# Reordering the work behind the last expert of a two-layer mixture of experts, and converting weights in the middle of a step

## The chip, the cores and the metric

The kernel runs on one core of a Trainium2 chip. The metric is the device time of one execution in microseconds (us). Matrix products run on TensorE (PE), copies out of PSUM and conversions on ScalarE (ACT) and VectorE (DVE), gathers and scatters are issued by GpSimd (POOL), and plain DMAs by SyncE (SP). Each engine works through its own instructions in order, and waits for others on semaphores.

## The reference

Three stages follow each other: attention with 4 sink keys and a window of 128, a first mixture of experts in which each of 1536 tokens goes to 2 of 8 experts, and a second one in which each token goes to one expert. Only the end of the first and the second are touched here:

```python
e_idx = np.argmax(logits, axis=1)          # logits = x @ w_gate + modality_bias[modality_id]
gate_w = probs[np.arange(N), e_idx]
for e in range(E):                         # E = 8 experts, N = 1536, D = 512, F = 1024
    mask = e_idx == e
    h = np.maximum(x[mask] @ w1[e], 0.0)
    out[mask] = gate_w[mask, None] * (h @ w2[e])
```

Everything is float32.

## The kernel before

**Precision.** Each float32 operand of the large products is split into a high part (written as fp32r) and a low part (the rest). ACT writes the high part by a copy, DVE the low part by a subtraction, and PE adds three products: high x high, high x low, low x high. The weights of an expert are 4 chunks of 128 x 2048 (1 MB each): chunks 0 and 1 are w1, 2 and 3 are w2. `split` has two slots for the two parts of an expert's weights.

**First layer, its end.** Expert 7 is the last of the first layer. Behind its products PE computes the scores of the second router for the tokens that expert 7 touches (`last_logits`, which needs yT of all four `y1_copy` of ACT), turns the output back to rows (`back`, 4 subtiles k = 0 to 3) and adds the scores to the tokens (`last_to_tokens`, which needs `last_share` of DVE). ACT scales the rows (`last_scale`), POOL scatters them (`scatter1`).

**Second router.** DVE picks each token's expert (`pick`), PE counts (`ranks(1)`), DVE places the tokens (`second_places`, `second_hots`), PE turns the places into lists of tokens (`codes2`), DVE reads them out (`second_sources`). `chosen_gate` on DVE, `coded_tiles(1)` and `coded_gates` on POOL, `slot_gates` on PE and again on DVE yield the gate of each row. `expert_order` writes the order in which experts are loaded, `tile_owners` and `fresh_tiles` which expert each tile has, and in which step new weights are to be converted (`todo`).

**Second layer.** Tokens are taken in tiles of 128. The most popular expert is known early, from 8 of the 12 blocks of 128 tokens: its weights come into `stage` (`popular_high`, `popular_low`, chunk by chunk), and tiles 0 and 1 are filled with its tokens, before the rest of the router is done. For tile t PE does `tx(t)` (turn x), `first(t, half)` twice (x @ w1), `th(t, half)` twice (turn h), and `second(t)` in two halves (h @ w2). ACT does `x_high`, `relu`, `h_high`; DVE `x_low`, `h_low`, and `y_copy` (times gate); POOL `gather` and `scatter`. A half of `first` or `second` is 8 matmuls of 512 columns with the high part of x or h, and 4 with the low part, which wait for `x_low` or `h_low` alone. `second_weights` converts the second expert; it comes through `raw`, loaded by SP when `order_ready` is 3.

**The loop.** From tile 3 on all engines go through `step(t)`: PE does first(t) with th(t-1) between, tx(t+1), second(t-1). `next_weights(t)` converts chunks 0 and 1 of the next expert in the first tile's step of an expert, and chunks 2 and 3 one step later. With these inputs the second layer has 14 tiles and 3 experts in use: tiles 0 to 6, tile 7, and tiles 8 to 13. Only steps 7 and 8 convert.

All order is written out by hand: the calls stand in each engine's program in the order in which it executes them.

## Time and profile before

| | us |
|---|---|
| median of 3 runs | 677.1 (675.16 to 678.22) |
| profiled execution | 675.41 |
| its span | 673.6 |
| PE busy in the span | 638.2 |
| PE busy from 463.7 us to the end of the span | 183.7 |
| PE's granted clock, mean over the span | 0.985 |

The span runs from the first to the last recorded instruction. A row of a timeline gives the start, the busy time, the engine, the line of the program, the operation, what it writes and reads, and in brackets how long the engine stood idle just before and what released it. "issue" means that the profile shows nothing that it waited for. A granted clock of 1.00 is 2.4 GHz, and 0.50 is 1.2 GHz. Busy matmuls overlap, so that the start of the next one, not the end of the last, tells the pace.

### The profile page before, as it was taken

The numbers are of one execution on the slowest core, as the hardware profiler recorded it, in microseconds if no ns is written. First come the engines' busy times: TensorE is split into PE (matmuls) and PEld (weight loads), VectorE is DVE, ScalarE is ACT, GpSimd is POOL, SyncE is SP. The second block draws the span as 40 slices with busy tenths as digits, with TensorE's granted clock in tenths as the row PEclk, the third lists the DMA queues.
The fourth block names the chain that finished last, engine by engine and source line by source line (L and its number), as shares of the span: only waits on it lengthen the run. The fifth ranks groups of instructions, "written<-read, shape, count | busy, mean of one in ns | idle before, by whom it ended". The sixth has DMA issues, their size and how long they took to land.

```text
span 673.6 us, 11243 instructions
## 1 busy us (share of the span) xinstructions
PE 638.2 (95%) x3866; PEld 580.5 (86%) x3867; DVE 328.5 (49%) x681; ACT 276.0 (41%) x529; POOL 185.1 (27%) x199
## 2 busy tenths in 40 slices
PE   7989999899999999999999999997989999999981
PEld 6989999898999999999999999986767888788861
DVE  4466645587465527263462624467767222542220
ACT  5668866442444234243433523234526123522110
POOL 2500100117361533516153241102542121121010
PEclk8999999999999999999999999999899999999996
DMA  7877822263684645646364510615549211011000
GB/s 209 280 245 245 284 71 73 70 245 79 231 231 132 139 128 157 190 145 165 108 127 161 156 20 12 162 63 172 157 165 369 92 48 47 20 33 47 16 32 11
DMA packets 51089, 89.84 MB, mean 133 GB/s; under 512 B 7919, under 2 KB 14063, under 8 KB 51040
## 3 DMA queue, kind: packets, MB, share of 16 engines
q1 hardware_dynamic: 41872, 69.21, 30.7%
q0 software_dynamic: 9168, 19.97, 13.4%
q8 instruction: 31, 0.51, 0.3%
q14 instruction: 18, 0.15, 0.1%
HBM read 73.13 MB, written 17.02 MB: 134 GB/s over the span
## 4 chain that ended last, share of the span: by engine, by line
PE 83%; DVE 6%; DMA 3%; issue 2%; ACT 2%; SPq 1%; POOL 0%; ACTq 0%; DVEq 0%; POOLq 0%
PE banks L1061 6%; PE banks L1060 6%; PE banks L1000 6%; PE banks L1079 6%; PE banks L1002 6%; PE banks L999 6%; PE banks L804 5%; PE banks L832 4%; PE banks L1343 4%; PE banks L1344 4%; PE banks L1348 4%; PE banks L1371 3%; PE banks L1372 3%; PE banks L1375 3%; PE banks L816 2%
## 5 line engine op out<-in xcount | busy, mean ns | idle before, releaser
L1825 DVE TENSOR_TENSOR split<-stage,split 128x2048 fp32r<-128x2048 f32 x32 | 73.3, 2290 | 41.6 <-ACT split L1455 41.4
L999 PE MATMUL banks<-xTs,split 128*128 128x416 f32 (+1 forms) x256 | 88.6, 350 | 0.0
L1000 PE MATMUL banks<-xTs,split 128*128 128x416 f32 (+1 forms) x256 | 86.4, 342 | 0.0
L651 POOL DMA_INDIRECT x_moe<-rows,dst_idx x25 | 49.3, 1971 | 113.2 <-DVE rows L2277 112.2
L1060 PE MATMUL banks<-hTs,split 128*128 128x416 f32 x224 | 79.9, 357 | 0.0
L1061 PE MATMUL banks<-hTs,split 128*128 128x416 f32 x224 | 78.6, 351 | 0.0
L1590 ACT ACTIVATE hTs<-banks 128x416 fp32r<-128x416 f32 x56 | 29.0, 518 | 81.5 <-PE banks L1002 81.5
L1455 ACT ACTIVATE split<-stage 128x2048 fp32r<-128x2048 f32 x32 | 61.0, 1908 | 0.7 <-DMA stage<-w1a 0.7
L1713 ACT ACTIVATE hTs<-banks 128x512 fp32r<-128x512 f32 x28 | 16.5, 597 | 105.3 <-PE banks L1358 105.3
L1002 PE MATMUL banks<-xTs,split 128*128 128x416 f32 (+1 forms) x256 | 56.2, 340 | 0.0
L1835 DVE CUSTOM_DVE_ANT_0 negs<-banks,masks 128x260 f32<-128x260 f32 (+2 forms) x96 | 34.9, 402 | 36.3 <-PE banks L804 35.1
L804 PE MATMUL banks<-k_sb,q_sb 128*128 128x260 f32 (+2 forms) x192 | 49.1, 380 | 3.6 <-DMA k_sb<-k_w 1.8
L1988 DVE SCALAR_TENSOR_TENSOR hTs<-banks,hTs 128x416 fp32r<-128x416 f32 x56 | 32.8, 587 | 38.7 <-ACT hTs L1590 38.7
L749 POOL DMA_INDIRECT out<-rows,dst x14 | 14.2, 1012 | 128.6 <-DVE rows L2430 111.5
L1343 PE MATMUL banks<-split,xTs 128*128 (+1 forms) x112 | 45.9, 410 | 3.6 <-issue 2.0
L1468 ACT ACTIVATE probs<-negs,negmax 128x260 f32<-128x260 f32 (+2 forms) x96 | 46.1, 484 | 7.2 <-DVE negmax L1835 7.2
L999 PEld LDWEIGHTS banks<-xTs,split 128*128 128x128 f32 x256 | 48.2, 188 | 0.7 <-issue 0.3
L1371 PE MATMUL banks<-split,hTs 128*128 (+1 forms) x112 | 45.3, 404 | 3.5 <-DVE rows L2430 1.8
L1000 PEld LDWEIGHTS banks<-xTs,split 128*128 128x128 f32 x256 | 48.2, 188 | 0.3
L1079 PE MATMUL banks<-hTs,split 128*128 128x416 f32 x224 | 48.0, 356 | 0.0
L2249 DVE TENSOR_TENSOR xTs<-banks,xTs 128x512 fp32r<-128x512 f32 (+1 forms) x28 | 16.4, 590 | 64.2 <-ACT xTs L1559 64.2
L1002 PEld LDWEIGHTS banks<-xTs,split 128*128 128x128 f32 x256 | 46.3, 188 | 0.3
(371 smaller groups left out, 1308.8 us busy)
## 6 DMA issues: line engine op xcount, KB each, us to landing
stage<-w1a SPq DMA_DIRECT2D x16, 1024.0 KB, 5.8
stage<-w2a SPq DMA_DIRECT2D x16, 1024.0 KB, 5.5
k_sb<-k_w SPq DMA_DIRECT2D x12, 520.0 KB, 4.8
raw<-w1b SPq DMA_DIRECT2D x4, 1024.0 KB, 6.4
raw<-w2b SPq DMA_DIRECT2D x4, 1024.0 KB, 9.5
q_sb<-q_t SPq DMA_DIRECT2D x24, 128.0 KB, 3.4
x_attention<-rows SPq DMA_DIRECT2D x12, 256.0 KB, 6.3
split<-x_moe SPq DMA_DIRECT2D x12, 256.0 KB, 3.7
```

The costliest lines, as they stand in the source:

```text
L651: pool.indirect_dma_start(out=x_dram[1], out_offset=rows_at(dst_idx[0], early_dst, e, k), in_=y_lines(e, k), in_offset=None, compute_op=AL ...
L804: mm = pe.matmul(S[:, j % 2, h, 0:n], q_sb[:, b, pair, h, :], k_sb[:, b, pair, 0:n], start=True, stop=True)
L999: pe.matmul(psum, piece(slot, 0, o + c * FH), xTs[:, 0, c, 0:cols], start=(c == 0), stop=False)
L1000: pe.matmul(psum, piece(slot, 1, o + c * FH), xTs[:, 0, c, 0:cols], start=False, stop=False)
L1002: mm = pe.matmul(psum, piece(slot, 0, o + c * FH), xTs[:, 1, c, 0:cols], start=False, stop=(c == DC - 1))
L1060: pe.matmul(psum, piece(e % 2, 0, o), hTs[:, 0, c, 0:cols], start=(c == 0), stop=False)
L1061: pe.matmul(psum, piece(e % 2, 1, o), hTs[:, 0, c, 0:cols], start=False, stop=False)
L1079: mm = pe.matmul(psum, piece(e % 2, 0, DC * F + c * D + d * P), hTs[:, 1, c, 0:cols], start=False, stop=(c == FC - 1))
L1343: pe.matmul(psH[:, half, :], xTs2[:, 0, c, :], weights(slot, 0, o), start=(c == 0), stop=False)
L1371: pe.matmul(psY, hTs2[:, 0, c, :], weights(slot, 0, o), start=(c == 0), stop=False)
L1455: act.activation(split_chunk(e % 2, 0, c), staged_chunk(e % 2, c), ACT.Copy).then_inc(high_done[c], 1)
L1825: dve.tensor_tensor(split_chunk(e % 2, 1, c), staged_chunk(e % 2, c), split_chunk(e % 2, 0, c).bitcast(F32), ALU.subtract).then_inc(low_do ...
```

## The change

One wait of SP goes, `codes2` moves into second(0), and the calls behind expert 7 stand in another order on PE, ACT and DVE. In the loop `next_weights(t)` stands between the two halves instead of at the end. No computation is added or left out.

```diff
@@ SP, load of the second expert
             sp.wait_ge(last_added, 1)
-            sp.wait_ge(gathered[0], 32)
             for c in range(CHUNKS):
@@ PE, second(t, e, slot)
-                        if isinstance(t, int) and t == 1 and half == 1:
-                            tx(2, 0, 2)
+                        if isinstance(t, int) and half == 1:
+                            if t == 0:
+                                codes2()
+                            elif t == 1:
+                                tx(2, 0, 2)
@@ PE, second_layer
                 tx(0, 0, 1)
                 back(last, 2, banks[:, 3, :])
+                first(0, 0, 0, 1)
                 back(last, 3, banks[:, 4, :])
-                first(0, 0, 0, 1)
-                ranks(1)
-                pe.wait_ge(scaled1, nth_sub(E, 0))
+                pe.wait_ge(scaled1, nth_sub(last, 0) + 1)
                 first(0, 1, 0, 1)
                 tx(1, 1, 1)
+                ranks(1)
                 first(1, 0, 0, 1)
+                pe.wait_ge(scaled1, nth_sub(E, 0))
                 th(0, 0)
                 first(1, 1, 0, 1)
-                codes2()
                 th(0, 1)
                 second(0, 0, 1)
                 slot_gates()
@@
-                e, slot = expert(2)
-                first(2, 0, e, slot)
-                first(2, 1, e, slot)
+                e2, slot2 = expert(2)
+                first(2, 0, e2, slot2)
+                first(2, 1, e2, slot2)
                 tx(3, 1, 2)
-                step(3, 1, 3)
+                th(2, 0)
+                e3, slot3 = expert(3)
+                first(3, 0, e3, slot3)
+                first(3, 1, e3, slot3)
+                th(2, 1)
+                tx(4, 0, 3)
+                second(2, e2, slot2)
@@ ACT, end of the first layer
                 turned_copy(2)
-                popular_high(0)
                 y1_copy(last, 3)
@@ ACT, step
                     h_high(t - 1, 0)
                     relu(t, 0)
+                    next_weights(t)
                     h_high(t - 1, 1)
                     relu(t, 1)
@@
-                    next_weights(t)
@@ DVE, step
                     h_low(t - 1, 0)
+                    next_weights(t)
                     h_low(t - 1, 1)
@@
-                    next_weights(t)
                     y_copy(t - 1, 1 - b, went)
@@ DVE, expert_phase
-                popular_low(0)
                 popular_first()
                 last_share()
-                popular_low(1)
+                popular_low(0)
                 late_scores()
                 all_scores()
+                x_low(0)
+                popular_low(1)
                 pick(noisy, 0, chosen[:], done_key)
...
-                x_low(0)
+                chosen_gate()
+                popular_low(2)
+                x_low(1)
                 second_places()
-                x_low(1)
-                chosen_gate()
                 second_hots()
-                popular_low(2)
-                second_sources()
                 h_low(0, 0)
                 popular_low(3)
+                second_sources()
                 h_low(0, 1)
+                slot_gates()
+                y_copy(0, 0, 0)
                 expert_order()
+                h_low(1, 0)
+                h_low(1, 1)
                 tile_owners()
                 fresh_tiles()
-                slot_gates()
-                y_copy(0, 0, 0)
-                h_low(1, 0)
-                h_low(1, 1)
                 x_low(2)
+                y_copy(1, 1, 0)
                 second_weights((0, 1))
-                y_copy(1, 1, 0)
                 x_low(3)
```

The start of ACT's part is shown by its instructions. On ACT, from the end of expert 7 on, before (`split<-stage1` is popular_high, `yT<-banks` y1_copy(last,3), `raw<-banks,sub_gate` last_scale, `xTs2<-banks` x_high, `rows<-banks` relu, `rc<-rb` the Exp):

```order
L1693 ACTIVATE split<-stage1 128x2048
L1596 ACTIVATE yT<-banks 128x416
L1693 ACTIVATE split<-stage1 128x2048
L1628 ACTIVATE raw<-banks,sub_gate 128x512 x2
L1702 ACTIVATE xTs2<-banks 128x512
L1628 ACTIVATE raw<-banks,sub_gate 128x512 x2
L1693 ACTIVATE split<-stage1 128x2048
L1708 ACTIVATE rows<-banks 128x512
L1693 ACTIVATE split<-stage1 128x2048
L1708 ACTIVATE rows<-banks 128x512
L1770 ACTIVATE rc<-rb 128x96
L1702 ACTIVATE xTs2<-banks 128x512
```

The same place of ACT now:

```order
L1604 ACTIVATE yT<-banks 128x416
L1700 ACTIVATE split<-stage1 128x2048 x2
L1636 ACTIVATE raw<-banks,sub_gate 128x512 x2
L1709 ACTIVATE xTs2<-banks 128x512
L1636 ACTIVATE raw<-banks,sub_gate 128x512
L1715 ACTIVATE rows<-banks 128x512
L1636 ACTIVATE raw<-banks,sub_gate 128x512
L1700 ACTIVATE split<-stage1 128x2048
L1776 ACTIVATE rc<-rb 128x96
L1715 ACTIVATE rows<-banks 128x512
L1709 ACTIVATE xTs2<-banks 128x512
L1700 ACTIVATE split<-stage1 128x2048
```

The copy of yT has moved ahead of the first popular_high, and x_high(1) ahead of the last one; between relu(0,0) and relu(0,1) stand now popular_high(2) and the Exp.

On DVE, around the gates of the rows, before (`used`, `tile_expert` end tile_owners, `last_used` to `todo` are fresh_tiles, the next three rows slot_gates, `rows<-banks,slot_gate` y_copy(0), `hTs` h_low(1,0) and (1,1)):

```order
L2118 TENSOR_SCALAR used<-noise_sb 128x1
L2119 CAST tile_expert<-owner_f 128x21
L2134 TENSOR_SCALAR last_used<-noise_sb 128x1
L2135 MEMSET shared 128x2
L2136 TENSOR_TENSOR shared<-owner_f 128x19
L2137 SCALAR_TENSOR_TENSOR shared<-owner_f,last_used,shared 128x19
L2139 SCALAR_TENSOR_TENSOR todo<-shared 128x20
L2202 COPY shared<-banks 128x63
L2204 TENSOR_TENSOR shared<-shared 128x21
L2205 TENSOR_TENSOR slot_gate<-shared 128x21
L2430 TENSOR_SCALAR rows<-banks,slot_gate 128x512
L2422 TENSOR_TENSOR hTs<-banks,hTs 128x512 x2
```

The same place of DVE now (`noise_sb<-pair_up_to` to `order` are expert_order):

```order
L2210 COPY shared<-banks 128x63
L2212 TENSOR_TENSOR shared<-shared 128x21
L2213 TENSOR_TENSOR slot_gate<-shared 128x21
L2438 TENSOR_SCALAR rows<-banks,slot_gate 128x512
L2110 TENSOR_REDUCE noise_sb<-pair_up_to 128x2
L2111 CAST used<-noise_sb 128x1
L2113 TENSOR_TENSOR noise_sb<-pair,iota_row 128x8
L2114 SCALAR_TENSOR_TENSOR pair_sq<-iota_row,pair_up_to 128x64
L2115 TENSOR_TENSOR pair_sq<-pair_sq,noise_sb 128x64
L2116 TENSOR_REDUCE order_f<-pair_sq 128x8
L2117 CAST order<-order_f 128x7
L2430 TENSOR_TENSOR hTs<-banks,hTs 128x512 x2
```

y_copy(0) now comes ahead of the order table, and the table ahead of h_low(1,0) and (1,1); the owners of the tiles come behind these.

## Rows read from the trace of the kernel before

**Rows 1.** The page: busy time of the engines in the whole span.
```profile
PE 638.2 (95%) x3866; PEld 580.5 (86%) x3867; DVE 328.5 (49%) x681; ACT 276.0 (41%) x529; POOL 185.1 (27%) x199
```

**Rows 2.** Timeline of PE to 483 us: start, busy, instruction, [idle before <-releaser].
```profile
466.26 1.06 PE L1139 MATMUL banks<-wg,yT 128*128 128x8 f32 x8 [1.62 <-ACT yT L1596]
...
470.44 1.44 PE L1149 MATMUL banks<-chosen,last_hot 128*128 128x24 bf16 x48 [1.75 <-DVEq L2344]
...
474.17 0.78 PE L1343 MATMUL banks<-split,xTs 128*128 128x512 f32 x1
...
482.85 0.47 PE L1343 MATMUL banks<-split,xTs 128*128 128x512 f32 x1 [0.96 <-issue]
```

**Rows 3.** Timeline of PE from 493 us to the step of tile 3.
```profile
493.99 0.50 PE L1371 MATMUL banks<-split,hTs 128*128 128x512 f32 x1 [1.00 <-DVE split L2408]
...
500.12 0.50 PE L1371 MATMUL banks<-split,hTs 128*128 128x512 f32 x1 [1.78 <-DVE rows L2430]
...
506.18 0.39 PE L1343 MATMUL banks<-split,xTs 128*128 x1
...
508.90 0.39 PE L1343 MATMUL banks<-split,xTs 128*128 x1
...
513.30 0.50 PE L1343 MATMUL banks<-split,xTs 128*128 x1 [1.08 <-issue]
```

**Rows 4.** Timeline of PE, steps of tiles 7 and 8.
```profile
572.20 0.39 PE L1371 MATMUL banks<-split,hTs 128*128 x1
...
576.66 0.49 PE L1343 MATMUL banks<-split,xTs 128*128 x1 [1.57 <-DVE split L1821]
```

**Rows 5.** Stretches: start:end, length, busy us (x instructions) per engine, clock, DMA share, GB/s.
```profile
470.00:475.50 5.50, 5.06 (x63) 4.90 (x64) 4.95 (x13) 2.22 (x4) 4.18 (x3) 0.50 0.88 299
```

**Rows 6.** Timeline of ACT behind expert 7.
```profile
463.89 1.91 ACT L1693 ACTIVATE split<-stage 128x2048 fp32r<-128x2048 f32 x1 [1.22 <-DMA stage<-w1b]
...
466.58 1.91 ACT L1693 ACTIVATE split<-stage 128x2048 fp32r<-128x2048 f32 x1 [0.38 <-DMA stage<-w1b]
468.40 1.25 ACT L1628 ACTIVATE raw<-banks,sub_gate 128x512 f32<-128x512 f32 x2
```

**Rows 7.** Timeline of SP: two loads of weights.
```profile
468.87 0.93 SPq L362 DMA_DIRECT2D stage<-w2b  x2
497.48 0.94 SPq L362 DMA_DIRECT2D raw<-w1b  x2
```

**Rows 8.** The tile stage, 455 to 500 us.
```profile
DMA to landing us min/median/max: 5.1/5.6/10.2
```

**Rows 9.** Timeline of DVE: the second router and y_copy(0).
```profile
478.30 0.26 DVE L2078 TENSOR_TENSOR counts<-banks,step 128x96 f32<-128x96 f32 x1 [1.59 <-PE banks L959]
...
481.28 0.42 DVE L2093 TENSOR_TENSOR xT<-tile_i,iota_row 128x252 f32<-128x252 int32 x1
...
484.26 1.77 DVE L2097 TENSOR_TENSOR row_hot<-row_i,iota_row 128x1536 bf16<-128x1536 int32 x1 [0.15 <-DVE gate L2241]
...
495.92 0.17 DVE L2109 CAST order<-order_f 128x7 int32<-128x7 f32 x1
...
499.31 0.75 DVE L2430 TENSOR_SCALAR rows<-banks,slot_gate 128x512 f32<-128x512 f32 x1
```

**Rows 10.** Timeline of ACT: chunk 1 of the second expert.
```profile
506.73 1.92 ACT L1450 ACTIVATE split<-raw 128x2048 fp32r<-128x2048 f32 x1 [0.71 <-DMA raw<-w1b]
```

**Rows 11.** Timeline of POOL.
```profile
484.50 1.60 POOL L716 TENSOR_TENSOR gate_rest<-gate,gate_parts 128x12 f32<-128x12 f32 x1
...
490.80 1.04 POOL L733 DMA_INDIRECT rows<-x_moe,src_idx  x1 [0.15 <-issue]
```

**Rows 12.** Timeline of ACT, the step of tile 7.
```profile
566.48 0.59 ACT L1708 ACTIVATE rows<-banks 128x512 f32<-128x512 f32 x1
...
571.54 3.72 ACT L1450 ACTIVATE split<-raw 128x2048 f32 x2 [0.77 <-issue]
```

**Rows 13.** Timeline of DVE, the step of tile 7.
```profile
573.84 4.49 DVE L1821 TENSOR_TENSOR split<-raw,split 128x2048 f32 x2 [2.35 <-ACT split L1450]
```

More of the change, by code:

```diff
@@ L1757, in second_weights @@
                         high_part(1, c)
+                popular_high(0)
                 popular_high(1)
@@ L1763, in expert_phase @@
                 last_scale(2)
+                relu(0, 0)
                 last_scale(3)
                 popular_high(2)
-                relu(0, 0)
-                popular_high(3)
-                relu(0, 1)
                 act.wait_ge(act_route, 6)
                 act.activation(rc[:], rb[:], ACT.Exp).then_inc(act_route, 1)
+                relu(0, 1)
                 x_high(1)
-                parted_tiles()
+                popular_high(3)
                 relu(1, 0)
                 h_high(0, 0)
+                parted_tiles()
                 relu(1, 1)
```

## The prediction, made before the result was known

> **What bounds the kernel now.** I read the page first, then PE's timeline behind 463.7 us, then the queues that its gaps point to. PE is busy 638.2 us of a span of 673.6 [rows 1], so time can only come from its gaps and from stretches at the lower clock. All edits act behind 463.7 us. There PE stands still 1.62 us for a copy of yT, 1.75 us for last_share, 0.96 us before first(1,0) [rows 2], 1.00 us for the low part of chunk 3, 1.78 us for y_copy(0), 1.08 us before first(3,0) [rows 3] and 1.57 us in the loop, before first(8,0) [rows 4]. From 470 to 475.5 us PE has a granted clock of 0.50 [rows 5], the 1.2 GHz level; it fell behind the first gaps.
>
> A half product (12 matmuls of 512 columns) takes 508.90 - 506.18 = 2.72 us at full clock [rows 3]: 1.8 for the first eight, 0.9 for the last four. Four transposes take some 0.35 us by PE's own order.
>
> **Up to first(0,0).** y1_copy(last,3) now goes ahead of popular_high(0), which held it from 463.89 for 1.91 us [rows 6]: the 1.62 us go. DVE does popular_first while PE is still busy and last_share ahead of popular_low(0), so the 1.75 us go as well. But PE doesn't keep that. ACT's second popular_high waits for its DMA until 466.58 in any order; 1.9 us for it and 1.25 for two last_scale end at 469.65 [rows 6], x_high(0) at 470.2, and first(0,0) starts at 470.3 instead of 474.17 [rows 2]: 3.9 us earlier, with a new wait of about 1.6 us in front.
>
> **Up to second(0).** If the clock stays at full, first(0,0), back(3), first(0,1), tx(1) and ranks end at 470.3 + 2.8 + 0.4 + 2.8 + 0.35 + 0.7 = 477.4. ACT has put popular_high(2), the Exp and relu(0,1) ahead of x_high(1). Chunk 2 is issued at 468.87 [rows 7] and lands after 5.6 us [rows 8], at 474.5; 1.9 + 0.2 + 0.5 + 0.6 later, at 477.7, first(1,0) starts instead of 482.85 [rows 2], 5.1 us earlier. Its last four matmuls wait for x_low(1), which stands on DVE behind chosen_gate (0.75) and popular_low(2) (2.2) from 476.6: 480.3, a new wait of 0.7. So th(0,0) comes at 481.2 and second(0) at 484.8, 4.8 us earlier. Its second half needs popular_low(3). On DVE 3.4 us of second_places (478.30 to 481.28 + 0.42), 1.8 of second_hots [rows 9], h_low(0,0) and the 2.2 of popular_low(3) follow on 480.2: 488.3, and the half starts there instead of 493.99 [rows 3], 5.6 us earlier. codes2 in the middle of second(0) costs nothing of its own, since it fills that wait. Chunk 3 lands 10.2 us after 469.4 [rows 7, 8], at 479.6, and is converted before relu(1,0) needs ACT at 481.8; up to 482 it is free.
>
> **Up to first(2,0).** slot_gates is reached at 491.4. y_copy(0) no longer stands behind expert_order, tile_owners and fresh_tiles: 0.65 us for the gates and 0.75 for the copy [rows 9] release second(1) at 493.5 instead of 500.12 [rows 3], 6.6 us earlier. h_low(1,0) stands behind expert_order and costs 0.4 of that. first(2,0) starts at 500.1 instead of 506.18: 6.1 us earlier.
>
> **The new wait.** This lead is not kept. The order table that releases the second expert's load is written at 495.92 + 0.17 = 496.1 before [rows 9], and at 493.4 + 1.7 = 495.1 now, one microsecond earlier. SP issued 1.4 us behind it, at 497.48 [rows 7], and ACT had chunk 1 at 506.73, 9.25 us after that [rows 10]. The removed wait on gathered[0] is worth nothing before, as that gather was issued at 490.80 [rows 11]; I take it at nothing (0 to 0.7 us, what it would have cost behind a table at 495.1). Now the issue is at 496.5, chunk 1 lands at 505.8, its conversion ends at 507.7, and behind it in ACT's queue stand relu(2,0), relu(2,1) and x_high(3). PE, which has th(2,0) behind tx(3), gets there at 505.9 and waits 2.4 us. first(3,0) starts at 509.5 instead of 513.30 [rows 3]. With th(2,0) already done, step 3 is 0.35 us shorter, of which I count 0.2: **-4.0 us** at first(4,0).
>
> **The loop.** Only tiles 7 and 8 convert in the loop. In step 7 ACT ends relu(7,0) at 567.1 and now converts there: 0.77 + 3.72 us [rows 12], to 571.6, h_high(6,1) to 572.1, just in time for the half at 572.20 [rows 4]. DVE's two low parts (4.49 us, [rows 13]) end at 574.3 and h_low(6,1) at 575.0, where PE's last four matmuls wanted it at 572.20 + 1.8 = 574.0: a wait of 0.95. It replaces the 1.57 (with its 0.2 of queue time, 0.75 gained). Step 8 has the same geometry and had no wait: 0.95 lost. Sum **+0.2 us**. Bounds: 0.75 + 0 if DVE gets in between, -0.8 us; twice the whole 4.49 without the 1.57, +7.4 us, if nothing covered a low part. I take +0.2, worked from the rows of this very step.
>
> **Sum.** -4.0 + 0.2 = -3.8 us on a profiled execution of 675.4 us (span 673.6): 671.6. That execution is 1.7 us under the median of 677.1 us, so the median comes to **673.3 us**.
>
> **A rule against it.** POOL's small subtractions took 1.60 us from 484.50 [rows 11], to 486.10, while DVE's row_hot ran from 484.26 to 486.03 [rows 9]. The change puts row_hot right behind the one-hots that POOL waits for, and popular_low(3) over its subtractions. By the rows I shift the end of coded_gates from 490.7 to 491.2, in time for slot_gates. The Trainium skill, SBUF — State Buffer, section "SBUF: two separate sides", says that a DVE operation with two SBUF inputs and a GpSimd operation that reads SBUF hold the shared ports in turn, each for its whole length. The trace agrees for the pair above, where the POOL operation ends 0.07 us behind the DVE one. With 0.1 to 0.5 us lost the rule leaves the sum as it is; where every POOL step meets a long DVE operation it gives the second rival below.
>
> **Rivals.**
> 1. The clock still falls (16%). For it: it fell once behind gaps of 1.62 and 1.75 us, and a gap of 1.6 stays. Against: the gaps of 1.00 and 1.78 us around 495 [rows 3] left it at full. If it is halved for 6.5 us behind 470, as before, the products end 3 us later, the order table with them: gain 0.8, 676.3 us.
> 2. POOL is held (12%). A third and fourth operation behind DVE, 2 us more, delays slot_gates and with it y_copy(0) and the order table by 1.4: 674.7 us.
> 3. The mid-step conversion costs nothing, or the load comes sooner (15%): first(8,0) 0.75 earlier and no loss in step 8, a gain of 4.8 to 5.5: 672.0 us.
> 4. Slower (9%): the second expert's chunk 1 is late. ACT's queue has the relu of tile 2 behind it, and PE now has th(2,0) directly behind tx(3), so each us of delay is one of the kernel's. It decides from a landing at 505.8 + 3.8 = 509.6 us on; 4 us beyond that, with the load sharing the engines with gathers and scatters that now come earlier, is 681 us. Against: the load before had the DMA engines just as full, and took 9.25 us.
>
> **Numbers.** The forecast has 48%, its own range is 672 to 675. A measurement of this kernel can tell about 0.5%, 3.4 us, so the line to faster is 673.7 us, 0.4 above the forecast. Of the forecast's 48, 30 lie beyond it and 18 within; the third rival adds 15 to faster, the first and second 28 to the same; the fourth 9 to slower. Faster 0.45, same 0.46, slower 0.09. The range for 8 in 10 reaches from the third rival to the first, with a us of the runs' own spread below: 670.8 to 677.0 us.
>
> **What would show it.** Right: no gap at last_logits(3); a wait of 1.6 us before first(0,0) near 470.3; clock at full through 470 to 476; first(2,0) near 500; a wait of over 2 us of th(2,0) for ACT behind chunk 1; first(3,0) near 509.5; in steps 7 and 8 waits of 0.95 us in front of the last four matmuls of second. Wrong: a clock of 0.50 behind 470, first(1,0) later than 479 (then chunk 2 was late), slot_gates waiting for POOL, or no wait at th(2,0), which would make it a gain of 6.

## The result, and the profile after

The changed kernel takes 679.43 us (median of 20 runs, 675.97 to 683.59), the kernel before 676.81 us on the same chip (20 runs). The ratio is 1.0039, 95% interval 1.0024 to 1.0055: slower by 0.4%, 2.6 us. I had forecast 673.3 us, a gain. The profiled execution took 679.85 us.

The page's busy time of PE, to set beside [rows 1]: the span is 677.9 us now instead of 673.6, and PE is busy 2.5 us more for the same products.

```profile
PE 640.7 (95%) x3866; PEld 579.3 (85%) x3867; DVE 329.9 (49%) x681; ACT 275.6 (41%) x529; POOL 185.1 (27%) x199
```

**Ahead of the loop.** PE's timeline after, to set beside [rows 2, 3]:

```profile
467.84 1.35 PE L1148 MATMUL banks<-chosen,last_hot 128*128 128x24 bf16 x48 [0.18 <-DVEq L2352]
...
471.08 0.47 PE L1342 MATMUL banks<-split,xTs 128*128 128x512 f32 x1 [0.97 <-ACT xTs L1709]
...
509.54 0.66 PE L1357 MATMUL banks<-ident,rows 128*128 128x128 f32 x4 [1.13 <-ACT rows L1715]
510.85 0.49 PE L1342 MATMUL banks<-split,xTs 128*128 x1 [0.66 <-ACT xTs L1709]
```

The 1.62 us for yT are gone and the 1.75 us before L1148 are 0.18. The new waits stand where they were forecast, but shorter: 0.97 us before first(0,0) instead of 1.6, 1.13 us before th(2,0) instead of 2.4. The executions differ before the change begins (by 0.76 us here), so I count from one mark in each: the start of the eight small products `banks<-early_moving,row_hot_popular`, at 461.88 us before and 462.64 after. From there first(4,0) starts after 63.87 us before and 60.13 after: **3.74 us gained**, where 4.0 were forecast.

**In the loop.** From first(4,0) to the end of the span it is 147.85 us before and 155.13 after: **7.28 us lost**, where 0.2 were forecast. All of it lies in the steps of tiles 7, 8 and 9, which last 14.03 + 12.42 + 12.40 = 38.85 us before and 15.57 + 16.63 + 14.11 = 46.31 after. PE's gaps there, after; before, the 1.57 us of [rows 4] was the only one over 0.25 us:

```profile
569.70 0.49 PE L1373 MATMUL banks<-split,hTs 128*128 x1 [0.32 <-ACT hTs L1720]
...
572.70 1.19 PE L1377 MATMUL banks<-split,hTs 128*128 x4 [0.92 <-DVE hTs L2430]
575.22 0.79 PE L1342 MATMUL banks<-split,xTs 128*128 x1 [1.33 <-issue]
...
586.77 0.49 PE L1373 MATMUL banks<-split,hTs 128*128 x1 [0.21 <-ACT hTs L1720]
...
589.83 1.19 PE L1377 MATMUL banks<-split,hTs 128*128 x4 [0.97 <-DVE hTs L2430]
591.85 0.67 PE L1342 MATMUL banks<-split,xTs 128*128 x1 [0.84 <-issue]
```

The two waits for DVE (L1377, the last four products of a second layer) are the 0.95 us that I forecast for each step, to within 0.03. What I did not forecast stands behind each: 1.33 and 0.84 us at the start of the next step that end in "issue", and in the column PEclk of the stretches (columns as in [rows 5]) the clock at its lower level:

```profile
574.00:576.00 2.00, 0.78 (x2) 0.69 (x3) 0.75 (x1) 0.00 (x0) 0.09 (x1) 0.73 0.00 0
576.00:578.00 2.00, 2.00 (x7) 1.52 (x6) 0.00 (x0) 0.00 (x0) 1.20 (x3) 0.50 0.11 38
578.00:580.00 2.00, 2.00 (x12) 1.63 (x11) 0.00 (x0) 0.00 (x0) 1.12 (x2) 0.91 0.19 47
...
593.00:595.00 2.00, 2.00 (x6) 1.54 (x6) 0.00 (x0) 0.00 (x0) 1.21 (x3) 0.50 0.03 3
```

The timelines of ACT and of DVE in step 7, to set beside [rows 12, 13]:

```profile
565.26 3.72 ACT L1458 ACTIVATE split<-raw 128x2048 f32 x2 [1.16 <-issue]
```

```profile
567.54 4.49 DVE L1829 TENSOR_TENSOR split<-raw,split 128x2048 f32 x2 [3.21 <-ACT split L1458]
571.96 0.68 DVE L2430 TENSOR_TENSOR hTs<-banks,hTs 128x512 fp32r<-128x512 f32 x1
```

The conversion ends on DVE at 572.0, and h_low(6,1) is queued behind it.

**POOL.** The two small casts of coded_gates, and what DVE did beside them:

```profile
485.08 1.71 POOL L711 CAST gate_parts<-gate 128x12 bf16<-128x12 f32 x1
...
487.69 2.14 POOL L717 CAST gate_parts<-gate_rest 128x12 bf16<-128x12 f32 x1
```

```profile
484.51 2.22 DVE L2105 TENSOR_TENSOR row_hot<-row_i,iota_row 128x1536 bf16<-128x1536 int32 x1
...
487.49 2.28 DVE L2416 TENSOR_TENSOR split<-stage,split 128x2048 fp32r<-128x2048 f32 x1
```

Each cast ends 0.06 us behind the DVE operation beside it, while a cast between the two takes 0.19 us. The pair of [rows 9, 11] showed the same. The Trainium skill, SBUF — State Buffer, section "SBUF: two separate sides", describes this as a port held for a whole instruction; the trace agrees. POOL's lost time cost the path nothing: slot_gates came at 493.63 us, 2.0 us behind the end of the last POOL operation that feeds it.

### The profile page after: what moved, and what is told of

It is laid out like the page before. It is cut to its first block, busy times and chain, and to the rows that moved or that the text cites. A ratio compares the mean times of both kernels' runs of the same rounds, so it can differ in the third digit from the quotient of the medians.

```text
span 677.9 us, 11238 instructions
## 1 busy us (share of the span) xinstructions
PE 640.7 (95%) x3866; PEld 579.3 (85%) x3867; DVE 329.9 (49%) x681; ACT 275.6 (41%) x529; POOL 185.1 (27%) x199
## 4 chain that ended last, share of the span: by engine, by line
PE 79%; DVE 7%; DMA 4%; issue 3%; ACT 3%; SPq 1%; POOL 0%; ACTq 0%; DVEq 0%; POOLq 0%
PE banks L1060 6%; PE banks L1059 6%; PE banks L1078 6%; PE banks L999 6%; PE banks L1001 6%; PE banks L998 6%; PE banks L803 5%; PE banks L831 4%; PE banks L1342 4%; PE banks L1377 4%; PE banks L1343 3%; PE banks L1347 3%; PE banks L1373 3%; PE banks L1374 3%; PE banks L815 2%
## 5 line engine op out<-in xcount | busy, mean ns | idle before, releaser
L1342 PE MATMUL banks<-split,xTs 128*128 (+1 forms) x112 | 47.3, 422 | 3.9 <-issue 2.2
L998 PEld LDWEIGHTS banks<-xTs,split 128*128 128x128 f32 x256 | 48.1, 188 | 0.8 <-issue 0.5
L999 PEld LDWEIGHTS banks<-xTs,split 128*128 128x128 f32 x256 | 48.2, 188 | 0.3
L2430 DVE TENSOR_TENSOR hTs<-banks,hTs 128x512 fp32r<-128x512 f32 x28 | 19.1, 689 | 57.3 <-ACT hTs L1720 56.9
```

Of the source, the lines that this page charges most:

```text
L998: pe.matmul(psum, piece(slot, 0, o + c * FH), xTs[:, 0, c, 0:cols], start=(c == 0), stop=False)
L999: pe.matmul(psum, piece(slot, 1, o + c * FH), xTs[:, 0, c, 0:cols], start=False, stop=False)
L1342: pe.matmul(psH[:, half, :], xTs2[:, 0, c, :], weights(slot, 0, o), start=(c == 0), stop=False)
```

## The experiments

Each ratio is to runs of the kernel before on the same chip. "Both at the end" is the changed kernel with the loop of before. e3, e5 to e8, e10, e13 and e15 edit the changed kernel; e4 and e9 edit "both at the end"; e2 and e11 edit the kernel before, and e12 takes part of the change out of "both at the end". The marks from the profiles, in us: "start" is from the mark named above to first(4,0), "7 to 9" the length of the three steps.

| kernel | ratio (95%) | start | 7 to 9 |
|---|---|---|---|
| before | | 63.87 | 38.85 |
| changed | 1.0039 (1.0024 to 1.0055) | 60.13 | 46.31 |
| e1 both at the end | 0.9942 (0.9923 to 0.9961) | 61.93 | 38.89 |
| e2 mid-step only | 1.0107 (1.0077 to 1.0136) | 64.14 | 43.30 |
| e3 ScalarE mid-step | 1.0004 (0.9982 to 1.0026) | 60.28 | 41.49 |
| e4 relu first | 0.9938 (0.9919 to 0.9958) | 59.42 | 38.89 |
| e5 split | 0.9950 (0.9924 to 0.9976) | 60.31 | 38.85 |
| e6 PE unrolled | 1.0005 (0.9981 to 1.0029) | 60.27 | 42.31 |
| e7 loads ahead | 0.9979 (0.9955 to 1.0002) | 60.22 | 40.72 |
| e8 filled, unrolled | 1.0004 (0.9978 to 1.0029) | 61.79 | 42.19 |
| e9 order first | 0.9949 (0.9916 to 0.9982) | 59.15 | 38.90 |
| e10 three together | 0.9899 (0.9862 to 0.9936) | 59.06 | 36.90 |
| e11 front only | 1.0026 (0.9987 to 1.0065) | 66.97 | 38.92 |
| e12 rest only | 1.0007 (0.9970 to 1.0043) | 64.55 | 38.84 |
| e13 filled loop | 1.0005 (0.9991 to 1.0018) | 60.52 | 43.69 |
| e14 changed again | 1.0027 (1.0011 to 1.0043) | 60.05 | 46.46 |
| e15 all four | 0.9882 (0.9863 to 0.9902) | 59.05 | 36.99 |
| e16 both at the end, again | 0.9947 (0.9926 to 0.9968) | 59.94 | 38.84 |

### Which part does it: e1 and e2

e1 takes the changed kernel and puts `next_weights(t)` back to the step's end; e2 takes the kernel before and makes the move alone (its DVE half is shown, ACT's is the same move):

```diff
                     h_low(t - 1, 0)
+                    next_weights(t)
                     h_low(t - 1, 1)
                     ...
-                    next_weights(t)
                     y_copy(t - 1, 1 - b, went)
```

> The changed kernel with one part taken back: the conversion of the next expert's weights stands at the end of a step again, on ScalarE and on VectorE. Everything ahead of the loop stays as changed. Theory (the loss is in the loop): the work ahead of the loop gained about 3.7 us and the mid-step conversion lost about 7.3 us, so this kernel takes about 672.9 us against 676.8 of before, ratio 0.994; step 7 lasts 14.0 us again, step 8 12.4, and no 0.50 stands in the granted clock of the steps 8 and 9. Rival (the loss lies in what the work ahead of the loop left behind, such as rows or weights that come later, and the loop merely shows it): steps 7 to 9 stay over 14 us and the ratio stays above 1.000.

> The kernel before with only the mid-step conversion added, on ScalarE and VectorE; the order ahead of the loop is that of before. Theory (the loss is in the loop): steps 7, 8 and 9 last about 15.6, 16.6 and 14.1 us as in the changed kernel, sum +7.3 us, so about 684 us, ratio 1.011. Rival (the two parts need each other): steps 7 to 9 sum to less than 41 us and the ratio is under 1.004.

672.25 and 683.15 us, where the kernel before took 676.17 on that chip: -3.9 and +7.0 us. The change is two changes of opposite sign, and they add up (3.1 us against the measured 2.6). Both rivals fall. e1's start is 61.93 instead of 60.13 because in that execution the clock was low from 510 to 515 us; e16, the same program, has 59.94. The profiled execution of e2 was the fastest of its six, with a mean granted clock of 0.988 where the other five had 0.979 to 0.986, and it holds something that the median doesn't: its steps 7 to 9 lost only 4.45 us, with the clock at full.

```profile
576.00:578.00 2.00, 0.98 (x4) 0.44 (x3) 0.98 (x2) 0.00 (x0) 0.00 (x0) 1.00 0.00 0
578.00:580.00 2.00, 1.69 (x7) 1.44 (x8) 0.09 (x1) 0.00 (x0) 1.00 (x2) 1.00 0.00 0
```

So 4.45 us are waits and gaps. Whether the rest is the clock is what e13 tests.

### Which engine: e3

In e3 only DVE's `next_weights(t)` goes back to the end.

> The changed kernel with VectorE's half of the conversion back at the end of a step, ScalarE's half left in the middle. Theory (VectorE's conversion holds the low parts of h, and with them the last four products of a second layer): those waits of 0.92 and 0.97 us are gone, and so are the empty starts of steps 8 and 9 and the low clock; what is left of ScalarE's is at most 0.3 us a step in front of the high parts of h, and the 1.57 us in front of first(8, 0) goes too, so 1 to 1.5 us under the kernel with both at the end. Rival (ScalarE's conversion does it): steps 7 to 9 stay at 15.6, 16.6 and 14.1 us, and the time stays near 679 us.

The time is 676.78 us, and neither theory holds: by the ratios e3 is 2.4 us under the changed kernel, but 4.2 over both at the end. The last four products don't wait any more. But what I took for a gain is a loss, as PE's and DVE's rows of step 7 show:

```profile
568.97 0.50 PE L1373 MATMUL banks<-split,hTs 128*128 x1 [0.32 <-ACT hTs L1720]
...
574.63 0.50 PE L1342 MATMUL banks<-split,xTs 128*128 x1 [2.67 <-DVE split L1829]
```

```profile
569.73 0.69 DVE L2424 TENSOR_TENSOR xTs<-banks,xTs 128x512 fp32r<-128x512 f32 x1 [0.28 <-ACT xTs L1709]
571.82 4.49 DVE L1829 TENSOR_TENSOR split<-raw,split 128x2048 f32 x2 [1.40 <-issue]
```

ACT converts before x_high(8), which starts 10.19 us into the step instead of e1's 7.54 (569.10 - 558.91, 568.44 - 560.90). DVE's x_low waits for it, DVE's conversion starts 1.7 us later than in e1 (12.91 us into the step instead of 11.20), and the wait before first(8,0) grows from 1.61 to 2.67 us. With the 0.32 us for h_high, ScalarE's half alone costs 2.6 us in the three steps of the profile (the ratios say 4.2, and what the other 1.6 are is not shown): an engine that converts early helps nothing where the next engine's piece stays last.

### The gap at a step's start: e6 and e7

e6 writes out TensorE's tiles 4 to 9; e7 moves the load of the expert number in it:

```diff
-                with pe.Fori(2, sure // 2 - 1) as r:
-                    step(r * 2, 0, r + 1)
-                    step(r * 2 + 1, 1, r + 2)
+                now, before = expert(4), (e3, slot3)
+                for t in range(4, sure - 2):
+                    first(t, 0, *now)
+                    ...
+                    after = expert(t + 1)
+                    second(t - 1, *before)
+                    now, before = after, now
```

> The changed kernel with TensorE's loop over the tiles 4 to 9 written out as straight code; each step still loads its two expert numbers at its start. It is the control for the next two. Both theories: as the changed kernel, within 1.5 us, 678 to 681 us; the gaps put down to nothing at the starts of steps 8 and 9 stay over 0.6 us each, since the loads of the expert numbers are still behind the wait, less what the branch at the loop's end had in them.

> The same straight code, but the expert number of the next tile is loaded ahead of the second layer of the step, and that of the tile before is kept in its register: one load a step instead of two, and none between the late low part of h and the next first product. Theory (the gap at a step's start is TensorE's sequencer, which is held at the late low part and has its loads still before it): the waits of 0.92 and 0.97 us stay, the gaps of 1.33 and 0.84 us go to under 0.4, and the clock stays at full more often: 2 to 4 us under the control. Rival (the gap is something else, such as the change of weights or the instructions being fetched): the gaps stay as in the control, and the times are equal within 1 us.

PE in steps 7 and 8 of e6, then of e7:

```profile
572.18 1.20 PE L1377 MATMUL banks<-split,hTs 128*128 x4 [0.91 <-DVE hTs L2429]
574.00 0.50 PE L1342 MATMUL banks<-split,xTs 128*128 x1 [0.63 <-issue]
...
587.16 1.20 PE L1377 MATMUL banks<-split,hTs 128*128 x4 [0.95 <-DVE hTs L2429]
588.96 0.50 PE L1342 MATMUL banks<-split,xTs 128*128 x1 [0.60 <-issue]
```

```profile
574.33 1.19 PE L1377 MATMUL banks<-split,hTs 128*128 x4 [0.87 <-DVE hTs L2437]
575.37 0.39 PE L1342 MATMUL banks<-split,xTs 128*128 x1
...
588.62 1.21 PE L1377 MATMUL banks<-split,hTs 128*128 x4 [0.95 <-DVE hTs L2437]
589.67 0.40 PE L1342 MATMUL banks<-split,xTs 128*128 x1
```

From the release of the last four products to the next first product it is 2.52 us in the changed kernel's step 7 (a new pass of the loop follows), 2.02 in step 8, 1.82 and 1.80 in e6, and 1.04 and 1.05 in e7, where the four products themselves fill 0.9. The waits for DVE stay. So the gap is PE's own instruction stream: held at the late semaphore, it has its two loads and the loop's branch still ahead of it, while otherwise these run under queued products. The loads cost 0.8 us (1.82 - 1.04), the loop 0.7 in the step that ends a pass of it (2.52 - 1.82) and 0.2 in the other (2.02 - 1.80), so that most of it, but not all, belongs to the branch. That is shown by the profiles; the medians agree (677.17 and 675.70 us, 1.5 apart where I had expected 2 to 4), but their intervals overlap. Part of what e7 saves goes back at once: its wait for h_high in step 8 is 0.46 us instead of e6's 0.23. I had set e6 within 1.5 us of the changed kernel; it came 2.3 under, which fits its profile, where no low clock stands in steps 7 to 9 (42.31 us) and the loop cost more than I thought.

### The clock: e8, e13 and e14

```diff
+                        if half == 1 and changed is not None:
+                            with pe.If(changed > 0):
+                                for k in range(4):
+                                    pe.matmul(banks[:, 7, :], hTs2[:, 0, 7, :], ..., start=True, stop=True)
                         pe.wait_ge(h_low_done, t * 2 + (half + 1))
```

`changed` is the difference of the two expert numbers, positive in steps 7 and 8 alone. e8 has the same four products in the straight code of e6, e14 is the changed kernel once more.

> The control with four products of 512 columns added in steps 7 and 8, in front of the wait for the low part of h; their result is used by nobody. Theory (part of the loss is the clock, which falls when TensorE is without work twice in a row): the products take the place of the 0.92 and 0.97 us of waiting, the gaps at the starts of the next steps stay, and the granted clock stays at 1.00 through steps 8 and 9: 1 to 3 us under the control. Rival (the clock plays no part in the mean of many runs): same as the control within 0.5 us, or slower by the products' 0.9 us a step where they don't fit the wait.

> The changed kernel, its loop left as it is, with four products of 512 columns in front of the wait for the low part of h in the steps in which the expert changes (7 and 8); their result is used by nobody. Theory (about 2 of the 6.6 us that the mid-step conversion costs are the clock, which falls behind the two idle stretches in a row; the rest are the waits and the empty starts): the waits of 0.92 and 0.97 us are filled, the gaps at the starts of steps 8 and 9 stay, the granted clock stays at 1.00 there, and the time is 1.5 to 2.5 us under the changed kernel of the same call. Rival (the clock has no part in the mean): within 0.5 us of it.

> The changed kernel once more, as the one to compare with in this call. Both theories: ratio to before 1.004, 95% within 1.001 to 1.007; its profile shows the waits of 0.9 us and the gaps of 1.3 and 0.8 us again. By the theory on the clock at least one of the two low stretches in steps 8 and 9 is there again; by its rival they are the exception and there is none.

e8 equals its control: there was nothing to save, since e6's profile holds no low clock in these steps (its gaps are 0.63 and 0.60 us instead of 1.33 and 0.84), and the median granted clock over the runs is 0.989 in both. In the kernel's own loop it is different. The stretches of e14, then of e13:

```profile
576.00:578.00 2.00, 1.86 (x4) 1.49 (x5) 0.00 (x0) 0.00 (x0) 1.19 (x2) 0.54 0.00 0
...
594.00:596.00 2.00, 2.00 (x6) 1.57 (x5) 0.00 (x0) 0.00 (x0) 1.21 (x2) 0.50 0.03 3
```

```profile
576.00:578.00 2.00, 0.97 (x4) 0.87 (x5) 0.75 (x1) 0.00 (x0) 0.29 (x1) 1.00 0.00 0
...
594.00:596.00 2.00, 2.00 (x13) 1.67 (x12) 0.00 (x0) 0.34 (x1) 1.21 (x3) 1.00 0.03 3
```

e13 keeps full clock, and PE's gaps in it are

```profile
577.03 0.49 PE L1342 MATMUL banks<-split,xTs 128*128 x1 [1.34 <-issue]
...
592.20 0.49 PE L1342 MATMUL banks<-split,xTs 128*128 x1 [0.84 <-issue]
...
605.14 0.50 PE L1342 MATMUL banks<-split,xTs 128*128 x1 [0.38 <-issue]
```

The waits in front of the last four products are filled, the gaps of 1.34 and 0.84 stay, and steps 7 to 9 take 43.69 us instead of 46.46, although a new gap of 0.38 us stands at the start of step 10. Two profiles of the changed kernel have both low stretches, at 3.0 and 3.2 us (46.31 and 46.46 against e2's 43.30). Over the runs the difference is less: 677.85 against 679.21 us, 1.4 us, where I expected 1.5 to 2.5. The intervals of the two ratios overlap, but both ratios share the runs of before; set against each other directly, the twelve runs of each kernel give 1.4 us with a 95% interval of 0.4 to 2.4 (bootstrap of the medians). The mean granted clock of every run points the same way: 0.979 to 0.989 in e14's twelve, 0.984 to 0.992 in e13's, seven of them above e14's highest. So the low clock has a share beyond the two profiles. Its size is less sure, since e2 and e6 kept full clock in their profiles without any filling, and e13's conditions brought their own 0.38 us.

### A smaller piece: e5

```diff
                     relu(t, 0)
-                    next_weights(t)
+                    next_weights(t, (0,))
                     ...
+                    next_weights(t, (1,))      # DVE likewise; (0,) is chunks 0 or 2, (1,) chunks 1 or 3
```

> The changed kernel with the mid-step conversion cut in two: one chunk of the pair between the halves, the other at the end of the step, on ScalarE and on VectorE. Theory (4.49 us of VectorE in one piece are too long for the place, a half of them is not): a low part of 2.25 us ends before the last four products want the low part of h, so neither wait of 0.92 and 0.97 us comes, nor the empty starts of steps 8 and 9; first(8, 0) needs only the chunk converted in the middle, so the 1.6 us in front of it go too. Steps 7 and 8 last 12.3 to 12.5 us each, and the time is about 1.6 us under the kernel with both conversions at the end: 670.6 us, ratio 0.992. Rival (any work in front of the second high part of h costs its length): steps 7 and 8 lose 1 us each, and the time is that of the kernel with both at the end or more.

The time is 672.76 us, not 670.6: by its ratio of 0.9950 it equals both at the end (0.9942 and 0.9947), as the rival had it. The steps last 13.37 and 12.98 us, 1.1 and 0.7 more than the 12.3 of a step that converts nothing. The rival's reason isn't there, though: PE waits neither for h_high nor for DVE. PE, and the low parts of h on DVE:

```profile
572.07 0.49 PE L1342 MATMUL banks<-split,xTs 128*128 x1 [0.91 <-issue]
...
585.05 0.49 PE L1342 MATMUL banks<-split,xTs 128*128 x1 [0.39 <-issue]
```

```profile
568.82 0.68 DVE L2431 TENSOR_TENSOR hTs<-banks,hTs 128x512 fp32r<-128x512 f32 x1
...
582.29 0.68 DVE L2431 TENSOR_TENSOR hTs<-banks,hTs 128x512 fp32r<-128x512 f32 x1
```

The low parts end at 569.50 and 582.97, just before PE's queue reaches the four products, so PE never stands still for them. Its instruction stream does: the next first product comes 2.57 and 2.08 us behind the release, the same as the 2.52 and 2.02 of the changed kernel. The price of a late semaphore starts 2.5 us ahead of the next product, before any wait shows. What e5 gains on the 1.57 us of [rows 4] it hands back so.

### Ahead of the loop: e4, e9, e11 and e12

Both on e1's kernel, e4 puts relu(2,0), relu(2,1), x_high(3) and x_low(3) ahead of chunk 1 of `second_weights`, and e9 moves one call on DVE; e11 is the kernel before with two moves, e12 is e1 without them:

```diff
@@ e9, DVE
+                expert_order()
                 slot_gates()
                 y_copy(0, 0, 0)
-                expert_order()
@@ e11, ACT and DVE
                 turned_copy(2)
-                popular_high(0)
                 y1_copy(last, 3)
                 ...
+                popular_high(0)
                 popular_high(1)
                 ...
-                popular_low(0)
                 popular_first()
                 last_share()
+                popular_low(0)
```

> The kernel with both conversions at the end of a step, and ahead of the loop relu(2, 0), relu(2, 1), x_high(3) and x_low(3) stand ahead of the conversion of chunk 1 of the second expert's second layer. Theory: the changed order waits about 1.1 us in front of th(2, 0) and 0.7 us in front of first(3, 0), for ScalarE, which at that time waits 1.45 us for the transfer of that chunk; with the short work ahead of it both waits go, and second(2), which needs the converted chunk, still finds it, since first(3) takes 3.6 us: 1 to 2 us under the kernel without this edit. Rival (the wait moves): second(2) waits for the chunks instead, and the time is the same within 0.3 us.

> The kernel with both conversions at the end of a step, and ahead of the loop expert_order stands ahead of slot_gates and y_copy(0) on VectorE, where the changed kernel leaves VectorE idle for 1.69 us. Theory (the waits of 1.13 us of th(2, 0) and 0.66 us of first(3, 0) come from the second expert's load, which waits for the order table): the table is written at about 494.3 instead of 497.2 us, the load is issued that much sooner, both waits go, and the time is 1.2 to 1.8 us under the kernel without this edit, near 670.8 us. Rival (the load is not bound by the table but by the DMA queue in front of it): chunk 1 lands when it did, the waits stay, and the time is the same within 0.3 us.

> The kernel before with two edits alone: on ScalarE y1_copy(last, 3) ahead of popular_high(0), on VectorE last_share ahead of popular_low(0). All else ahead of the loop, and the loop, as before. Theory (the gain ahead of the loop is mostly the two gaps of 1.62 and 1.75 us behind expert 7): TensorE's first product of the second layer comes 3 us sooner and most of this lasts to the loop, 2 to 3.5 us under before, ratio 0.995 to 0.997. Rival (the lead is lost again at y_copy(0), which stands behind the tables, and at the second expert): under 1 us of gain, ratio over 0.9985.

> The kernel with both conversions at the end of a step, with the same two edits taken back: y1_copy(last, 3) behind popular_high(0), last_share behind popular_low(0). What is left of the change is the order from first(0, 0) on. Theory: the gaps of 1.6 and 1.75 us come back, and the gain left is that of y_copy(0) ahead of the tables and of th(2, 0) ahead of first(3): 1 to 2 us under before, ratio 0.997 to 0.999. Rival (each part alone brings the same): the whole 3.9 us stay, ratio 0.994.

e4 and e9 remove the wait of th(2,0): their starts are 59.42 and 59.15 us against 59.94 to 60.31 in seven of the ten profiles of the unedited order, 0.5 to 0.9 and 0.8 to 1.2 us less; the other three (60.52, 61.79 and 61.93) have a low clock behind 470 or 511 us. That is under what the medians can tell (672.27 and, on a chip where all runs spread more, ratio 0.9949), so it is shown by the profiles alone, and e9's 1.2 to 1.8 was too much. The wait before first(3,0) goes in neither: it is 0.66 us for ACT in e9 and 0.64 us that end in "issue" in e4. And in e4 part of the wait moves, as its rival had it: step 3 lasts 12.55 us instead of 11.92, with 0.35 us of waiting for h_low, which stands behind three conversions of DVE now instead of two. In e9 the table ends where DVE had been idle, at 505.60 + 0.17, 0.36 us ahead of the gates:

```profile
505.60 0.17 DVE L2117 CAST order<-order_f 128x7 int32<-128x7 f32 x1
506.13 0.23 DVE L2210 COPY shared<-banks 128x63 f32<-128x63 f32 x1 [0.36 <-PE banks L1399]
```

The results of e11 and e12 were not expected. In the profiles the front moves alone lose 3.1 us up to first(4,0) and the rest alone 0.7; together they gain 3.7. The ratios, 1.0026 and 1.0007, don't tell either from no change, but they exclude my 2 to 3.5 us for e11 and the rival's whole gain for e12. PE and DVE in e11:

```profile
472.40 0.47 PE L1343 MATMUL banks<-split,xTs 128*128 128x512 f32 x1 [0.41 <-ACT xTs L1701]
...
477.80 2.08 PE L1348 MATMUL banks<-split,xTs 128*128 128x512 f32 x4 [3.30 <-DVE xTs L2416]
```

```profile
469.23 4.49 DVE L2408 TENSOR_TENSOR split<-stage,split 128x2048 fp32r<-128x2048 f32 x2 [0.15 <-DVE chosen L2343]
...
477.05 0.69 DVE L2416 TENSOR_TENSOR xTs<-banks,xTs 128x512 fp32r<-128x512 f32 x1 [0.15 <-DVE rb L2473]
```

first(0,0) starts 8.32 us behind the mark, as in the changed kernel, but x_low(0) still stands behind two popular_low of 4.49 us and the whole of pick: PE waits 3.30 us, and its clock then is 0.50 from 478 to 483 (and once more from 504 to 508). So the front moves seem to need the change's move of x_low(0) to a place ahead of popular_low(1) and pick; this is read from the trace, and no run makes that move alone. In e12 the two gaps are back (1.70 and 1.67 us), and so is the low clock behind them.

### Together: e10, e15 and e16

> Three edits together on the changed kernel: one chunk converted in the middle of a step and one at its end, TensorE's tiles 4 to 9 as straight code with the expert number loaded ahead of the second layer, and expert_order ahead of slot_gates. Theory: steps 7 and 8 last 12.4 us each, 1.7 us less than with both conversions at the end, and the load of the second expert gives 1.2 to 1.8 more: near 669 us, ratio 0.990. Rival (the three work on the same wait): no faster than the best of them alone, 0.994.

> The kernel with the three edits together, and relu(2, 0), relu(2, 1), x_high(3) and x_low(3) ahead of chunk 1 of the second expert as well. Theory (both remove the same wait for the second expert's load): no more than 0.3 us between it and the three alone, ratio 0.990. Rival (each has a wait of its own): another 0.7 us, ratio 0.989.

> The kernel with both conversions at the end of a step once more, as the other one to compare with in this call: ratio to before 0.994, 6.6 us under the changed kernel; no low clock in steps 7 to 9.

e10 has e5, e7 and e9 on the changed kernel. No gap over 0.15 us is left in steps 7 and 8; each lasts 12.3 us, the length of a step that converts nothing:

```profile
574.36 0.39 PE L1342 MATMUL banks<-split,xTs 128*128 x1
...
586.66 0.39 PE L1342 MATMUL banks<-split,xTs 128*128 x1
```

The ratio is 0.9899, as forecast, so the gains at the load and in the loop add up. e15 has e4's moves too: 669.65 us against 677.41, 0.9882 (0.9863 to 0.9902), the lowest ratio of the study, though the interval overlaps e10's. Its start is e10's (59.05 and 59.06), which fits two edits that remove one and the same wait; but e10's profile has a low clock from 472 to 476 us that e15's has not, and e15 gives 0.6 us back in step 3 (12.52 us instead of 11.94). e16 repeats e1: 0.9947, 5.4 us under e14 where 6.6 was expected, with the clock at full in steps 7 to 9.

## Why the prediction was wrong

**The term ahead of the loop was right in size, partly by luck.** -4.0 forecast; -3.74 in the profile, -3.9 and -3.6 us by the ratios of e1 and e16. Its steps: first(0,0) 3.9 earlier, measured 3.85; first(1,0) 5.1, measured 5.1; full clock from 470 to 475.5, measured 1.00. first(2,0) was to be 6.1 earlier and was 4.6. slot_gates came at 492.87 (493.63 less the executions' 0.76) instead of 491.4: popular_low(3) was 0.8 us late, 0.45 of it behind a row_hot of 2.22 us instead of 1.77, and PE waited 0.65 us for h_low(0,1) behind second_sources, which I had not counted. This did no harm, as the lead was to be lost at th(2,0) anyway: its wait was 1.13 us instead of 2.4. The order table, forecast 1 us earlier than before, came 0.4 later (497.22 - 0.76 = 496.46), and SP issued the load at 497.82 instead of 496.5; ACT had chunk 1 at 506.33, 0.5 behind the forecast, because the load took 8.5 us instead of 9.25. That error and the shorter load offset each other in part. first(3,0) came 3.2 us earlier instead of 3.8, and the rest came back in step 3, which is 0.5 us shorter (11.92 instead of 12.45), where I counted 0.2.

**The term for the loop was wrong: +0.2 forecast, +7.3 in the profile, +5.4 and +6.6 us by the ratios (changed against both at the end).** The step that failed is "It replaces the 1.57 (with its 0.2 of queue time, 0.75 gained). Step 8 has the same geometry and had no wait: 0.95 lost." The length of the wait came out (0.92 and 0.97 us), with luck in it: PE reached the four products and DVE ended h_low(6,1) both some 0.6 us later than forecast (12.99 us into the step instead of 12.37 for DVE). But I took a wait's length for its price. PE's instruction stream is in order too, and the loads of expert numbers and the loop's branch, which in the kernel before ran ahead under queued products, came out behind it. I had also put h_high(6,1) "just in time", at no cost, and PE waits 0.32 and 0.21 us for it. By the profiles the 7.5 us of steps 7 to 9 divide so: 3.0 the clock (changed against e2), 1.0 the loop, mostly its branch (e2 against e6), 1.6 the loads (e6 against e7), and 1.9 what the waits for DVE and ACT cost beyond the 1.57 us that went (e7 against before). That last part alone is more than the whole +0.2. From start to start of the products, against 0.23 us for each in a full queue, e7 loses 1.03 and 1.11 us at the waits for DVE, 0.47 and 0.62 at the waits for ACT and 0.25 just behind, against 1.73 us at the gap that went. Over the runs the clock is nearer 1.4 (e13), which gives 5.9 us, between the 5.4 and 7.0 of the comparisons.

**The clock.** I had a rival for it, but at 470 us, where it stayed at full in both profiles of the changed kernel. (The profiles of e1, e3 and e5 have 0.50 from 467 to 471 us and that of e13 from 470 to 474, and first(1,0) came up to 0.5 us later for it; the 3 us of the rival came in none.) In the loop I did not ask; a single gap of 1.57 us had left it at 1.00 there. Two gaps with only four products between them, 0.92 and 1.33 us in step 7 and 0.97 and 0.84 in step 8, were followed by 0.50.

**The range and the chances.** I named +7.4 us as the loop's upper bound and then took none of it into the range, which ended at 677.0. That the profile came so near this bound is chance: the bound was two full conversions of 4.49 us less 1.57, and the waits for DVE are 0.92 and 0.97. The only slower case (9%) was another mechanism, ahead of the loop, which didn't come. A term whose bounds were -0.8 and +7.4 should have moved chance to slower.

## What to carry to other kernels

In this kernel a wait late in a loop's step cost its length and, behind it, the register loads and the branch that it stopped from running ahead; look at what the sequencer has to do between the wait and the next product, and load such numbers before the wait. A long conversion may be moved into a step only in pieces that end before the next short operation on the same engine is due, and every engine of the chain has to be moved, not the first one alone; even then PE's instruction stream has to be clear behind it, as e5 and e10 show (38.85 and 36.90 us). When a change has a part with near bounds and one with far bounds, try them apart: here one was worth -3.9 us and the other +7.

## What was not expected of the hardware

Two idle stretches with four products between them (0.92 and 1.33 us, 0.97 and 0.84 us) were each followed by about 3 us at a granted clock of 0.50, in both profiles of the changed kernel. The same stretches in e2's profile (0.90 and 1.32, 0.97 and 0.80) were not, so it isn't certain in each execution. Low stretches came in single profiles at 8, 52 and 164 us too, far ahead of all that the edits touch; they make single profiles differ by more than many edits are worth, which is why the marks are counted from behind them.

An operation of DVE can be the longer one too. In the 15 profiles with the changed order row_hot starts together with POOL's `moving` (0.61 us) and takes 2.22 us; in the three with the order of before (before, e2, e11) `moving` is done earlier and row_hot takes 1.77, although a longer POOL operation starts behind it. This fits DVE standing back for the POOL operation that was there with it; no run parts the two alone.
